# A fused attention and MLP kernel: attention on pairs of heads with block-diagonal queries, no bias pass, and the MLP's weights split later

## What is computed

```python
# q, k, v: [4, 8, 576, 64]   s: [4, 8, 576]
scores = matmul(q, k.T) / sqrt(64)
cum    = cumsum(maximum(s, 0), axis=-1)
bias   = -(cum[:, :, :, None] - cum[:, :, None, :])          # row i, key j: cum_j - cum_i
scores = where(causal, -1e9, scores + minimum(bias, 0))
attn   = exp(scores - max(scores)); attn = attn / (sum(attn) + 1e-9)
x = matmul(attn, v)                                          # -> [2304 tokens, 512]
h = x @ w_in;  x = (h * cos(h)) @ w_out                      # 512 -> 2048 -> 512
xn = x / sqrt(mean(x*x) + 1e-6) * rms_g
out = (silu(xn @ w_gate) * (xn @ w_val)) @ w_out2            # 512 -> 1536 -> 512
```

## Time and profile before

| what | value |
|---|---|
| device time, median of 3 runs | 1217.87 us (1214.45 to 1220.16) |
| span of the profiled execution, first to last instruction | 1214.9 us |
| mean granted TensorE clock | 0.996 |
| busy: PE, PEld, DVE, ACT, POOL | 98%, 90%, 61%, 51%, 29% |
| attention, until the first matmul of B | 322.7 us |
| first matmul of `down` | 330.7 us |

### The profile page before, as it was taken

How to read it: one execution, slowest core, us unless ns; L and a number is a source line. 1 busy time by engine, 2 the same in 40 slices (tenths; PEclk the granted TensorE clock), 3 DMA queues, 4 the chain that set the end, 5 groups by cost and what they waited for, 6 DMA issues and landing times.

```text
span 1214.9 us, 25276 instructions
## 1 busy us (share of the span) xinstructions
PE 1186.0 (98%) x8511; PEld 1098.9 (90%) x8511; DVE 745.1 (61%) x1826; ACT 622.2 (51%) x1554; POOL 354.8 (29%) x473
## 2 busy tenths in 40 slices
PE   6999999999999999999999997999999999999998
PEld 4888888888899999999999897999999999999997
DVE  7989898988785555655556687534344444443432
ACT  4788777877656555655556463223323322332221
POOL 6788888877760000000000399200000000000000
PEclk9999999999999999999999999999999999999999
DMA  5333343332230000000000044000000000000000
GB/s 125 86 91 95 87 102 93 82 97 62 72 102 1 1 2 1 0 0 0 0 0 0 28 122 123 17 19 1 17 17 0 17 0 17 17 0 17 0 18 18
DMA packets 91393, 46.94 MB, mean 39 GB/s; under 512 B 60816, under 2 KB 81296, under 8 KB 91344
## 3 DMA queue, kind: packets, MB, share of 16 engines
q1 hardware_dynamic: 91344, 46.31, 13.9%
HBM read 41.49 MB, written 4.79 MB: 38 GB/s over the span
## 4 chain that ended last, share of the span: by engine, by line
PE 89%; DVE 6%; ACT 2%; issue 2%; POOL 0%; DMA 0%; SPq 0%; DVEq 0%; POOLq 0%; ACTq 0%
PE psum L1259 26%; PE psum L1215 14%; PE psum L1166 14%; PE psum L1271 12%; PE psum L1152 7%; PE psum L1131 6%; PE psum L1102 6%; PE psum L1085 4%; DVE b_r L808 2%; DVE b_lo L819 1%; PE psum L1107 1%; DVE b_r L805 1%; ACT b_c L548 1%; ACT b_r L545 1%; DVE b_g L814 0%
## 5 line engine op out<-in xcount | busy, mean ns | idle before, releaser
L1259 PEld LDWEIGHTS psum<-c_x,cw 128*128 128x128 f32 x2592 | 322.8, 191 | 7.1
L1259 PE MATMUL psum<-c_x,cw 128*128 128x256 f32 x2592 | 326.5, 283 | 0.0
L1215 PE MATMUL psum<-b_hi,wout 128*128 128x288 f32 x1024 | 227.1, 297 | 11.7 <-DVE b_lo L819 11.7
L1215 PEld LDWEIGHTS psum<-b_hi,wout 128*128 128x128 f32 x1024 | 171.9, 189 | 14.2 <-DVE b_lo L819 13.7
L905 DVE TENSOR_TENSOR c_t<-psum,c_t 128x256 f32<-128x256 f32 x108 | 45.9, 425 | 191.7 <-ACT c_t L651 191.7
L1215 PE MATMUL psum<-b_lo,wout 128*128 128x288 f32 x512 | 151.2, 295 | 0.0
L651 ACT ACTIVATE c_t<-psum 128x256 f32<-128x256 f32 x108 | 41.5, 384 | 207.7 <-PE psum L1259 207.6
L1271 PE MATMUL psum<-cw,c_hi 128*128 128x512 f32 x432 | 135.2, 394 | 0.0
L1042 POOL TENSOR_SCALAR cw<-stage 128x512 fp32r<-128x512 f32 x36 | 26.8, 745 | 333.5 <-PE psum L1166 323.4
L1152 PE MATMUL psum<-pT_hi,vs 128*128 128x320 f32 (+3 forms) x448 | 113.5, 312 | 0.0
L1166 PE MATMUL psum<-bx_odd,win 128*128 128x288 f32 x768 | 112.8, 295 | 0.2 <-ACT c_rms L572 0.2
(11 more groups left out here) (108 smaller groups left out, 2054.6 us busy)
## 6 DMA issues: line engine op xcount, KB each, us to landing
cum_row<-cum_rows SPq DMA_DIRECT2D x32, 288.0 KB, 3.4
stage<-in_moe_w_out SPq DMA_DIRECT2D x28, 256.0 KB, 2.6
out<-stage SPq DMA_DIRECT2D x18, 256.0 KB, 2.1
raw_q<-in_q SPq DMA_DIRECT2D x32, 128.0 KB, 2.2
raw_k<-in_k SPq DMA_DIRECT2D x32, 128.0 KB, 2.3
raw_v<-in_v SPq DMA_DIRECT2D x32, 128.0 KB, 2.3
stage<-in_moe_w_in SPq DMA_DIRECT2D x16, 256.0 KB, 2.6
stage<-in_moe_w_gate SPq DMA_DIRECT2D x12, 256.0 KB, 2.8
```

Of the source, the lines that this page charges most:

```text
L1215: last = mm(Y_BANKS[f][:, 0:TB], wout[j][:, a, cols], g[j % 4][:], start=(j == 0 and m == 0), stop=(j == NJ - 1 and m == 2))
L1259: last = mm(GV_BANKS[c % 3][:, n * TC:(n + 1) * TC], weights(c, a)[:, kc], c_x[:, b, kc], start=(kc == 0 and m == 0), stop=(kc == KC - 1 a ...
```

## The change

- **Pairs of heads.** Attention goes over 16 pairs, written out in 17 steps (pair p together with what is left of pair p-1) on every engine, with no loop and no deeper pipeline. The host lays out k transposed for the two heads above each other (128 rows), and q transposed in nine tiles of 64 queries as 128x128 blocks that are zero off the diagonal, so TensorE's 18 transposes a pair of q and k and their copies go. `scores` has nine tiles a pair, each in three passes (128 rows are 64 queries of two heads), with a 64-column mask matmul.
- **No bias pass.** `cum8` (the cum rows of the two heads, broadcast to 64 rows each) is added in `logits`; `make_bias` is gone. `cum8` of pair 0 is computed in place from `s_first`; the others come through memory as before.
- **One buffer** of probabilities `prob` in place of two, two psum banks of scores in place of four. `prob_T` transposes 25 blocks of 128x128 a pair, in units of 5, 8, 6 and 6, straight after the exponent.
- **Two-pass PV.** `times_v(p, a)` has [v_hi | v_lo] of one head as its 128 weight columns and pT_hi and pT_lo as its two moving operands: 12 matmuls a head. Rows 0-63 and 64-127 of the result are added afterwards: ACT copies one half to `x_part` (`copy_part`), DVE adds the other (`add_parts`).
- **x scaled at the end.** The inverse sums go to memory and back as broadcast rows (`turn_inverse`, four transfers on SP and a wait between them), and POOL multiplies 128x576 of x (`normalise`).
- **Weights.** Pieces are contiguous in memory. Only 6 pieces are split in attention and 2 at its end by POOL; the other 24 of `w_in` and `w_out` go in B's first tile, two a chunk, `hi` by ACT (`tile_piece`) and `lo` by POOL. The last pair's first three ups are placed between its units and its `times_v`.

The core of the diff (the part with `if now` is DVE's step p):

```diff
-            def make_bias(h, par, nth):
-                ...
-                nc.vector.tensor_scalar(bias[(par + nth) % 2][0:r, 0:w], cum_row[par][0:r, 0:w], col, col,
-                                        ALU.min, ALU.subtract).then_inc(bias_ready, 1)
+            def scores(p, n):
+                ...
+                at_least(pe, logits_ready, QT * p + (n - 1 if n >= 2 else n))
+                ...
+                    for m, (a, k) in enumerate(((0, 0), (0, 1), (1, 0))):
+                        mm(psum[:, b, 0:hi - lo], src[:, a, at:at + P], src[:, k, lo:hi],
+                           start=(m == 0), stop=(m == 2 and not diag))
+            def prob_T(p, u):
+                at_least(pe, pT_lo_ready, 4 * p + u - 1)
+                at_least(pe, exp_done, QT * p + TILE.index(TILES_OF[u][-1]) + 1)
+            def times_v(p, a):
+                at_least(pe, pT_lo_ready, 4 * p + 4)
+                at_least(pe, v_lo, p + 1)
+                at_least(pe, x_added, 2 * p + a)
+            def evac_hi(p, u):
+                at_least(act, probT_done, 4 * p + u + 1)
+                at_least(act, pv_done, 2 * p)
+                for src, dst in unit_moves(u, pT_hi):
+                    last = nc.scalar.copy(dst, src)
+            def logits(p, n):
+                ...
+                at_least(dve, scores_done, QT * p + n + 1)
+                if p >= 1:
+                    at_least(dve, probT_done, 4 * (p - 1) + UNIT_OF[i] + 1)
+                if now:
+                    logits(p, 0)
+                if before:
+                    evac_lo(p - 1, 2)
+                    sum_plus_eps(p - 1)
+                if now:
+                    logits(p, 1)
+                if before:
+                    row_inverse(p - 1)
+                    evac_lo(p - 1, 3)
+                if now:
+                    logits(p, 2)
+                    logits(p, 3)
+                if before:
+                    add_parts(p - 1, 0)
+                if now:
+                    logits(p, 4)
+                    logits(p, 5)
+                    evac_lo(p, 0)
+                if before:
+                    add_parts(p - 1, 1)
+                if now:
+                    logits(p, 6)
+                    evac_lo(p, 1)
+                    logits(p, 7)
+                    logits(p, 8)
+            def turn_inverse(p):
+                at_least(sp, inv_ready, p + 1)
+                ...
+                sp.wait_ge(inv_stored, 32 * (p + 1))
+                ...
+                    sp.dma_start(inv_row[p % 2][HALF_ROWS[a], :],
+                                 inv_dram[2 * p + a:2 * p + a + 1, :].to_broadcast([64, SEQ])).then_inc(inv_loaded[p % 2], 16)
+            def tile_piece(j, half):
+                n = OWN_PIECES + 2 * j + half
+                ...
+                piece_hi(n)
```

More of the change, by code:

```diff
@@ L35 @@
 NC2 = FF2 // P
[L38 to L48, removed]
+NP = NH // 2
+QT = SEQ // HD
+TILE = [QT - 1 - n for n in range(QT)]
+KEYS = [HD * (i + 1) for i in range(QT)]
+BLOCKS = [i // 2 + 1 for i in range(QT)]
+P_AT = [P * sum(BLOCKS[:i]) for i in range(QT)]
+P_COLS = P * sum(BLOCKS)
+HALF8 = 288
+QK_COLS = SEQ + QT * P
+NKB = 5
+V_COLS = NKB * P
+PAIR_COLS = QK_COLS + V_COLS
+PT_ROW = 896
+PT_AT = P
+PT_COLS = PT_AT + 4 * PT_ROW + QT * P
+FIRST_QK = SEQ + 2 * P
 TB = 288
@@ L90, in sem @@
             return ctx.enter_context(nc.semaphore(name))
+        EARLY = 4
+        pieces = [("in", j) for j in range(EARLY)]
+        for j in range(NJ):
+            pieces.append(("out1", j))
+            if j + EARLY < NJ:
+                pieces.append(("in", j + EARLY))
+        N_B = len(pieces)
+        for c in range(NC2):
+            pieces += [("gate", c), ("val", c), ("out2", c)]
+        NPIECES = len(pieces)
+        NUMBER = {piece: n for n, piece in enumerate(pieces)}
         xT = sb("xT", [P, KC, TOKENS], F32)
@@ L419, in _ @@
-            run_steps(sp, step)
-            sp.wait_ge(in_lo, NJ)
-            for n in range(NPIECES):
+            for p in range(NP):
+                if 1 <= p and p + 1 < NP:
+                    load_cum(p + 1)
+                if p >= 1:
+                    turn_inverse(p - 1)
+                if p + 3 < NP:
+                    load_qk(p + 3)
+                    load_v(p + 3)
+                if 1 <= p <= IN_ATTENTION:
+                    load_piece(p - 1)
+            for n in range(IN_ATTENTION, IN_ATTENTION + 3):
+                load_piece(n)
@@ L422, in _ @@
+            turn_inverse(NP - 1)
+            for n in range(IN_ATTENTION + 3, NPIECES):
                 load_piece(n)
@@ L1195, in _ @@
-            run_steps(pe, step)
+            for p in range(NP + 1):
+                now, before = p < NP, p >= 1
+                if now:
+                    scores(p, 0)
+                if before:
+                    prob_T(p - 1, 2)
+                if now:
+                    scores(p, 1)
+                else:
+                    pe.wait_ge(bx_lo, 1)
+                    pe.wait_ge(logits_ready, QT * NP)
+                    up(0, 0, 0)
+                if before:
+                    prob_T(p - 1, 3)
+                if now:
+                    scores(p, 2)
+                    scores(p, 3)
+                else:
+                    up(1, 1, 0)
+                if before:
+                    times_v(p - 1, 0)
+                if now:
+                    scores(p, 4)
+                    prob_T(p, 0)
+                    scores(p, 5)
+                else:
+                    up(2, 2, 0)
+                if before:
+                    times_v(p - 1, 1)
+                if now:
+                    scores(p, 6)
+                    prob_T(p, 1)
+                    scores(p, 7)
+                    scores(p, 8)
```

919 lines of the change are left out of this document (407 added, 512 removed).

## The result

| what | before | changed |
|---|---|---|
| device time, median | 1217.77 us (1214.45 to 1220.16) | 1268.37 us (1267.64 to 1272.53) |
| ratio, 95% interval | | 1.0427 (1.0404 to 1.0449) |
| span of the profiled execution | 1214.9 us | 1266.2 us |
| first matmul of B | 322.7 us | 357.1 us |
| first matmul of `down` | 330.7 us | 374.4 us |

What follows compares the result with a forecast made beforehand. TensorE bounds attention now (18.9 us a pair); after the change, waits in written order would (19.0). Attention's ends -6.1, B's first tile +3.3, clock +10: +7 on the 1217.87 median gives 1225 us, range 1196 to 1243.

Steps and rivals of the forecast that it cites:

- the one through the engines: Attention: waits in written order among ACT, DVE and TensorE, with handoffs, close a chain of 19.0 us a pair.
- A cost bounded by a row in the other direction (a load for a store): Attention's inverse transfer: a 2 KB load in 4-byte elements lands in 3.0 us, against 8 us available; costs nothing.

Runs made afterwards that it cites:

- e_contig: Changed kernel with only the row inverses' store rewritten as 128 runs of 9 values, not 1152 single values: 1243.0 us, 1.0202 of before.
- order_c: Changed kernel with written orders putting a pair's tail beside the next's head, and the inverse loaded and used three pairs behind: 1187.6 us, 0.9755 of before.
- order_c_contig: order_c with the store of the inverses as 128 runs of 9 values: 1126.8 us.
- e_fill: Changed kernel plus 39 TensorE matmuls of zeros a pair in attention, where TensorE waits for DVE: 1282.1 us.

## What to carry to other kernels

When a change cuts an engine's work, look for every closed chain through written orders, transfers and back, not only the one through the engines: walk each queue that a new transfer's wait holds up, and what stands behind it there. A cost bounded by a row in the other direction (a load for a store) has no upper bound yet; say so in the range. If a new small store scatters single values, turn them on chip first: here one transpose of 0.3 us turned a store of 1152 single values into one of 18 runs. The old one had held SP for some 8 us and delayed what was issued behind it. And work out the written order as carefully as the instructions: nearly the same instructions gave 22.2, 20.4, 17.1 and 13.0 us a pair, depending on their order and the form of one store.

## What the runs showed of the hardware

- **A store of single 4-byte values holds its queue.** 1152 values, 4.6 KB, kept SP waiting 8.4 us on average; the same bytes in 128 runs landed in 1.8 us (e_contig). Whether it is the number of the runs or their distance in memory was not tried apart. Loads of 144 KB issued behind such a store landed in 10.1 us (order_c), behind one in runs in 3.2 (order_c_contig).
- **DVE waits out a POOL instruction even for nine columns.** Both forms of the sum, with all their operands in SBUF, did; `pT_lo`, with one operand in psum, kept 1.22 us for 1024 columns in the changed kernel and all its variants.
- **A longer TensorE program can cost in a loop elsewhere.** With the fillers in attention, the step from the last chunk of B's tiles 2 and 4 to the next one (`down` to `down`) took 6.2 to 7.5 us in place of 3.2 in all five such kernels, and the chunk behind it up to 5.7. Just there TensorE's loop, two tiles long, jumps back. In e_fill's trace (weight loads, then one-microsecond stretches with the columns of the stretches above) TensorE waits for nothing that the profile shows, and then runs at half clock for some six us:

```profile
537.83 0.50 PEld L1119 LDWEIGHTS psum<-bx_odd,w 128*128 128x128 f32 x2 [1.99 <-issue]
```

```profile
536.00:537.00 1.00, 0.08 (x1) 0.00 (x0) 0.38 (x1) 0.55 (x2) 0.00 (x0) 1.00 0.00 0
...
538.00:539.00 1.00, 1.00 (x5) 1.00 (x6) 0.00 (x0) 0.28 (x1) 0.00 (x0) 0.50 0.00 0
```

The page of e_fill has 55 transfers of instructions, that of the changed kernel 32:

```profile
q8 instruction: 55, 0.90, 0.4%
```

The Trainium skill ("Runtime: NRT & Kernel Launch", section "Instruction fetch mechanics") says that a taken branch whose target is outside the window of two pages held on chip stops the engine for a fetch. The row agrees with that, but that it is the cause was not tried apart.
